# Fused attention, gated layer and gated convolution on one core: a new up operand, a new issue order and work for GpSimd

## The reference

```python
w = softmax(weight_gen, axis=-1)                      # 8 heads, 7 taps
x = sum_k w[..., k] * x_padded[s + k]                 # causal window of 7 tokens, per head of 24 channels
# layer 1
xk = mu_k * x + (1 - mu_k) * x_prev;  xr = mu_r * x + (1 - mu_r) * x_prev
v = relu(xk @ w_k) ** 2 @ w_v                         # 192 -> 1024 -> 192
y = sigmoid(xr @ w_r) * v
# layer 2
h = relu(y @ w_in)                                    # 192 -> 1024
c = conv_w[0] * h[s-1] + conv_w[1] * h[s] + conv_w[2] * h[s+1]
out = (h * sigmoid(c)) @ w_out                        # 1024 -> 192
```

## Time and profile before

| | us |
|---|---|
| median of 3 runs | 737.31 |
| profiled execution, whole | 737.71 |
| its span, first to last instruction | 735.9 |
| PE busy | 696.3 (95%) |
| DVE busy | 681.4 (93%) |
| ACT busy | 648.5 (88%) |
| POOL busy | 3.6 |

### The profile page before, as it was taken

One profiled execution on the slowest core, in us unless ns is written; L12 is line 12 of the kernel. 1 busy time (PEld: TensorE's weight loads), 2 busy tenths in 40 slices (PEclk: granted clock), 3 DMA queues, 4 the chain that ended last, 5 costly groups with the idle time before them and its releaser, 6 DMA issues.

```text
span 735.9 us, 10798 instructions
## 1 busy us (share of the span) xinstructions
PE 696.3 (95%) x3531; PEld 590.7 (80%) x3531; DVE 681.4 (93%) x1057; ACT 648.5 (88%) x1351; POOL 3.6 (0%) x9
## 2 busy tenths in 40 slices
PE   0788999999999999999999999999999999999995
PEld 0677988888888888888888887888888888888984
DVE  7999999999999999998999999999999999786776
ACT  3788999899989989898989889898998989897985
POOL 1000000000000000000000000000000000000000
PEclk9999999999999999999999999999999999999999
DMA  6701101010102001010101101010200101000000
GB/s 157 231 16 40 55 12 54 16 55 22 54 1 71 5 22 55 22 53 23 55 1 28 48 23 53 23 54 0 76 1 23 54 22 44 22 1 1 22 23 21
DMA packets 9053, 28.76 MB, mean 39 GB/s; under 512 B 1038, under 2 KB 4136, under 8 KB 8870
## 3 DMA queue, kind: packets, MB, share of 16 engines
q1 hardware_dynamic: 8840, 28.05, 11.6%
q10 hardware_dynamic: 158, 0.03, 0.0%
HBM read 21.69 MB, written 6.39 MB: 38 GB/s over the span
## 4 chain that ended last, share of the span: by engine, by line
PE 75%; DVE 18%; issue 4%; ACT 1%; DMA 1%; SPq 0%; DVEq 0%; ACTq 0%
PE up L320 32%; PE od L436 20%; PE dn L384 4%; PE dn L400 4%; PE dn L407 4%; PE dn L404 4%; PE dn L403 4%; DVE att L830 3%; PE dn L406 3%; DVE prod L818 3%; DVE cv L927 3%; DVE cv L937 2%; PE mid L291 1%; DVE kq_lo L894 1%; DVE gat L946 1%
## 5 line engine op out<-in xcount | busy, mean ns | idle before, releaser
L436 PE MATMUL od<-wo_sb,gat 128*128 128x192 f32 x1040 | 188.9, 329 | 6.4 <-DVE gat L946 6.3
L436 PEld LDWEIGHTS od<-wo_sb,gat 128*128 128x128 f32 x1040 | 173.8, 191 | 17.7 <-DVE gat L946 5.4
L927 DVE SCALAR_TENSOR_TENSOR cv<-h,prm,cv 128x512 f32<-128x512 f32 (+2 forms) x144 | 98.4, 693 | 19.9 <-ACT cv L606 19.7
L894 DVE TENSOR_TENSOR kq_lo<-ksq,kq_hi 128x512 fp32r<-128x512 f32 (+2 forms) x144 | 89.3, 632 | 14.3 <-ACT kq_hi L572 13.8
L937 DVE SCALAR_TENSOR_TENSOR cv<-h,prm,cv 128x512 f32<-128x512 f32 (+2 forms) x144 | 98.3, 693 | 0.4
L606 ACT ACTIVATE cv<-h,prm 128x512 f32<-128x512 f32 (+2 forms) x144 | 97.0, 675 | 0.0
L818 DVE TENSOR_TENSOR prod<-xin,wgt 128x768 f32<-128x768 f32 (+2 forms) x108 | 95.6, 886 | 1.0
L830 DVE TENSOR_TENSOR att<-att,prod 128x768 f32<-128x768 f32 (+2 forms) x108 | 95.4, 883 | 0.0
L946 DVE TENSOR_TENSOR gat<-h,cv 128x512 f32<-128x512 f32 (+2 forms) x144 | 90.6, 631 | 0.4 <-ACT cv L613 0.2
L597 ACT ACTIVATE h<-up 128x512 f32<-128x512 f32 (+2 forms) x144 | 79.9, 556 | 11.3 <-PE up L320 10.0
L613 ACT ACTIVATE cv<-cv 128x512 f32<-128x512 f32 (+2 forms) x144 | 83.7, 584 | 6.0 <-DVE cv L937 5.3
(11 more groups left out here) (111 smaller groups left out, 1351.6 us busy)
## 6 DMA issues: line engine op xcount, KB each, us to landing
xin<-in_x SPq DMA_DIRECT2D x14, 960.0 KB, 4.7
out<-o_sb SPq DMA_DIRECT2D x14, 384.0 KB, 2.3
wgt<-in_weight_gen SPq DMA_DIRECT2D x1, 1288.0 KB, 6.2
h<-in_moe_w_v SPq DMA_DIRECT2D x1, 768.0 KB, 4.5
wo_sb<-in_moe_w_out SPq DMA_DIRECT2D x1, 768.0 KB, 8.0
xin<-in_x SPq DMA_DIRECT2D x1, 768.0 KB, 4.1
h<-in_moe_w_k SPq DMA_DIRECT2D x1, 512.0 KB, 5.1
h<-in_moe_w_k SPq DMA_DIRECT2D x2, 256.0 KB, 5.6
```

The source lines that it names most:

```text
L436: mm = nc.tensor.matmul(o, lhs, wo_sb[:, c, :], start=(c == 0 and b % 2 == 0), stop=(c == NC - 1), skip_group_check=(b % 2 == 1))
L894: nc.vector.tensor_tensor(ring(kq_lo, c, n), ring(ksq, c, n), ring(kq_hi, c, n).bitcast(F32), ALU.subtract).then_inc(kql_ok, 1)
L927: nc.vector.scalar_tensor_tensor(o, win(w, c, -1), prm[:, 3 + c:4 + c], o, ALU.mult, ALU.add)\
```

## The change

- **Second up layer.** `small_copy`, `add_small`, the shift matrix and the tile `small` are gone. The weights `wr` are now 256 columns wide, with channels 128 to 191 twice, so `r_part` gives the gate in both halves of `dn1`, and `y_mult` multiplies both halves (128 rows instead of 64). `y_hi_part` has a third instruction: part 2 casts all 128 rows into `y2_s`, part 3 casts rows 0 to 63 into `y2_t`, whose rows 64 to 127 get the low part of the upper half. The fourth product of `up2` takes `y2_s`, the fifth `y2_t`; rows 64 to 127 of the weights repeat rows 0 to 63 (in `wi2_lo` they hold a cast of the weight itself), and the product sums the halves.
- **Softmax** in four parts of 448, 672, 1120 and 1456 elements. In parts 1 to 3 GpSimd does the difference and the product; DVE keeps maximum, sum, plus 1e-9 and reciprocal.
- **GpSimd** makes the low parts of `w_in` (1024 columns at a time) and the wrapped columns at the end, by halves of the chunks.
- **Ends.** Slot 0 and the last slot are apart: window NG-1 takes the last slot too and has three slots, window NG has one. ACT leaves out `carry` of window NG-1.
- **Loads.** `w_r` is loaded with six DMAs instead of three, and the softmax weights of part 1 are loaded ahead of `w_in`.
- **Order.** `step(i)` is written anew on PE, ACT and DVE; the numbers of the arguments say nothing, since each engine has its own offset.

```diff
-            nc.gpsimd.memset(small[0:D2, :].bitcast(F32), 0.0).then_inc(small_zero, 1)
+            def split_wi(n):
+                rows = (P, D2)[n]
+                pool.wait_ge(w_cast, 3 + n)
+                nc.gpsimd.tensor_tensor((wi_lo, wi2_lo)[n][0:rows, :], raw_w(2 + n, 0, rows),
+                                        (wi_hi, wi2_hi)[n][0:rows, :].bitcast(F32), ALU.subtract).then_inc(wi_split, 1)
+            def softmax_differences(n):
+                lo, hi = SM_PARTS[n]
+                pool.wait_ge(sm_max, n)
+                nc.gpsimd.tensor_tensor(wgt_rows(lo, hi), wgt_rows(lo, hi), vals(hi - lo)[1], ALU.subtract)\
+                    .then_inc(sm_sub, 1)
+            def softmax_quotients(n):
+                lo, hi = SM_PARTS[n]
+                pool.wait_ge(sm_exp, n + 1)
+                pool.wait_ge(sm_rec, n)
+                nc.gpsimd.tensor_tensor(wgt_rows(lo, hi), wgt_rows(lo, hi), vals(hi - lo)[1], ALU.mult).then_inc(sm_ok, 1)
+            for n in range(2):
+                half = slice(n * HALF, (n + 1) * HALF)
+                pool.wait_ge(h_free, NC * n_windows(NG - 1) - (HALF if n == 0 else 0))
+                nc.gpsimd.memset(h3[:, half, AFTER + PPB - 1:AFTER + P:PPB], 0.0).then_inc(wrap_fix, 1)
+                nc.gpsimd.tensor_copy(part_of(half, AFTER, 0), part_of(half, ALONE, 1)).then_inc(h_wrap, 1)
...
-                terms = ((w_hi, a_hi), (w_lo, a_hi), (w_hi, a_lo), (w2_hi, a2), (w2_lo, a2))
+                terms = ((w_hi, a_hi), (w_lo, a_hi), (w_hi, a_lo), (w2_hi, a2), (w2_lo, b2))
...
-            def add_small(g):
...
-                nc.tensor.matmul(dn[1][0:D2, 0:n], shift[:, :], small[:, 0:n], start=False, stop=True,
-                                 skip_group_check=True)\
-                  .then_inc(sum_done, 1)
...
-                    nc.scalar.activation(y2_s[0:D2, 0:n], y2[:, 0:n], ACT.Copy).then_inc(yhi_ok, 1)
+                    o, rows = (y2_s, P) if part == 2 else (y2_t, D2)
+                    nc.scalar.activation(o[0:rows, 0:n], y2[0:rows, 0:n], ACT.Copy).then_inc(yhi_ok, 1)
...
-        SM_ENDS = [0, FIRST[3] + 1, FIRST[6] + 1, FIRST[9] + 1, FIRST[13] + 1, TPP + 1]
+        SM_ENDS = [0, FIRST[3] + 1, FIRST[6] + 1, FIRST[11] + 1, TPP + 1]
...
-            dve.wait_ge(h_free, NC * n_windows(NG))
-            dve.wait_ge(h_keep, NC)
-            nc.vector.tensor_copy(h3[:, :, 2 * P:3 * P - 1], h3[:, :, KEEP + P + 1:KEEP + 2 * P]).then_inc(h_wrap, 1)
-            nc.vector.tensor_copy(h3[:, :, KEEP + 1:KEEP + P], h3[:, :, P:2 * P - 1]).then_inc(h_wrap, 1)
```

More of the change, by code:

```diff
@@ L526, in xr_hi_part @@
                     nc.scalar.activation(xr2_s[D2:P, 0:n], xkr2[D2:P, 0:n], ACT.Copy).then_inc(xrhi_ok, 1)
-            def small_copy(g):
-                if not group(g):
-                    return
-                act.wait_ge(d_done, NC * g + NC)
-                if not eq(g, 0):
-                    act.wait_ge(sum_done, g)
-                n = size(g) * P
-                nc.scalar.activation(small[D2:P, 0:n], dn[1][D2:P, 0:n], ACT.Copy).then_inc(small_ok, 1)
             def y_hi_part(g, part):
@@ L633, in carry @@
             def carry(w, c):
-                if not window(w):
+                if not window(w) or eq(w, NG - 1):
                     return
@@ L771, in _ @@
+                z_carry(i - 6)
+                k_relu(i - 6, 0)
+                first_tap(i - 7, 4)
+                gate_sigmoid(i - 7, 1)
+                k_square(i - 6, 0)
+                k_relu(i - 6, 1)
+                k_cast(i - 6, 0)
+                k_relu(i - 6, 2)
+                o_copy(i - 8, 0)
+                if i == 6:
+                    cast_wv()
+                o_copy(i - 8, 1)
+                k_square(i - 6, 1)
+            for i in range(3, NG + 9):
                 step(i)
-            act.wait_ge(wrap_fix, 2)
+            act.wait_ge(h_keep, NC)
@@ new lines, in step @@
+                if i == 6:
+                    split_wk(1)
+                k_lo(i - 6, 0)
+                conv_after(i - 7, 3)
+                att_add(i - 5, 2)
+                att_mult(i - 5, 4)
+                k_lo(i - 6, 1)
+                conv_before(i - 7, 4)
+                k_lo(i - 6, 2)
+                if i == 6:
+                    split_wv()
+                att_add(i - 5, 3)
+                gate(i - 7, 1)
+                att_mult(i - 5, 5)
+                att_mult(i - 5, 6)
@@ new lines, in step @@
+                k_lo(i - 6, 3)
+                softmax_front(i - 3)
+                conv_after(i - 7, 4)
+                k_lo(i - 6, 4)
+                gate(i - 7, 2)
+                conv_before(i - 7, 5)
+                att_add(i - 5, 4)
+                k_lo(i - 6, 5)
+                gate(i - 7, 3)
+                att_add(i - 5, 5)
+                k_lo(i - 6, 6)
+                if i == 5:
+                    params()
+                k_lo(i - 6, 7)
+                gate(i - 7, 4)
+                conv_before(i - 7, 6)
@@ new lines, in step @@
+                att_add(i - 5, TAPS - 1)
+                conv_after(i - 7, 5)
+                y_mult(i - 6, 1)
+                y_mult(i - 6, 2)
+                conv_after(i - 7, 6)
+                if i == 5:
+                    split_wk(0)
+                y_lo_part(i - 6, 1)
+                y_lo_part(i - 6, 2)
+                conv_before(i - 7, 7)
+                att_mult(i - 4, 0)
+                gate(i - 7, 5)
+                conv_after(i - 7, 7)
+                att_mult(i - 4, 1)
```

491 lines of the change are left out of this document (229 added, 262 removed).

## The result

The changed kernel takes 745.25 us (median of 4 runs, 744.3 to 746.02); the kernel before, run beside it, 737.32. The ratio is 1.011, with a 95% interval of 1.009 to 1.0122. The forecast was 728.5 us with a range of 723 to 745: the sign was wrong, and the time lies just above the range. The profiled execution has a span of 742.5 us, 6.6 more than before; it was the shortest of the four runs (744.3), so the traces show 1.3 us less of the loss than the medians.

The account below looks back on a forecast made before the run. PE was taken to bound 12 to 14 of 18 groups, DVE the start, a DVE and ACT chain the end. From 737.7 us, -3.7 - 1.6 - 2.3 - 1.5 = -9.1 gave 728.6; forecast 728.5, range 723 to 745.

Parts of the forecast that it names:

- Step 5: GpSimd's own time: eight operations of 7.7 to 23 us in all, taken to cost nothing beside DVE's work.
- Rival A: Start and middle: DVE stands still while GpSimd reads SBUF, so the moved work comes back on DVE; 742 us, chance 0.3.
- step 2: Softmax in the middle groups: a group absorbs about 4.8 us, and 0.3 us of stall is left; -1.6 us.
- Step 3: The start: DVE is rid of 4.3 us of work, against a later arrival of `w_in`; -2.3 us.
- The walk: The start's new DVE order gone through with old spacings: last low part of y of group 1 ends at 59.0.
- step 4: The end: 33.4 against 32.5 us, but two `down2` chunks behind the last `down1` bring it 2.6 earlier; -1.5 us.
- The wait of 3 us for `kq_hi`: The start: DVE was to wait about 3 us near 32, with ACT's casts of `w_in` ahead of k chunks.
- Step 1: `add_small` goes: a shorter PE in all 18 groups by product spacing, with 0 taken for stalls; -3.7 us.
- B: All groups: the new order stalls PE, y half a microsecond late in 14 groups; 735.5 us, chance 0.12.
- C: The start brings nothing, `w_in` late and the order no better, its term +2; 733 us, chance 0.08.

Follow-up runs that it names:

- experiment 6: The kernel before with `add_small` removed and `w_r` loaded by six DMAs, old order, everything on DVE: 737.27 us, 0.9998 of the kernel before.
- experiment 1: The changed kernel with all of GpSimd's arithmetic (softmax and the split of `w_in`) back on DVE, end copies left on GpSimd: 739.76 us, 1.0026 of the kernel before.
- experiment 2: The changed kernel with only the softmax differences and quotients back on DVE, the split of `w_in` left on GpSimd: 741.5 us, 1.0058 of the kernel before.
- experiments 4 and 7: The changed kernel with GpSimd's arithmetic on DVE and five softmax parts, 735.39 us; that kernel with 11 additional GpSimd instructions of 768 elements, 734.72 us, single run.

## Why the prediction was wrong, by its steps

**Step 5 failed:** "Beside DVE's work they cost nothing in this sum." In its place the traces show 15.7 us in which DVE stood still, for work that takes DVE itself 10.1, and the medians show 5.5 us more than with that work on DVE. It was also what the forecast stood on: with GpSimd at nothing, DVE is 10 us lighter. Rival A had this mechanism, its place in the start and the middle, and its sign, and 742 us for the time; it got 0.3 because no row showed the two engines together. The missing row was no evidence against it. That A comes so near the time is in part luck: it stood on the same 4.8 us of step 2, and took off 2.4 us for a wait of DVE that did not come. Its range is also worked out a little wide: by its own terms 0.9, 2.2 and 2.7 ns give 734.3, 745.4 and 749.7 us, where the text has 733.5, 746 and 751. GpSimd's rate was inside the bounds: 2.0 to 2.2 ns an element for the quotients (1456 in 3.02 us), up to 2.6 for the splits, 20.3 us for all where the page GPSIMD Engine Reference of the Trainium skill (Performance versus the Vector engine) led to an estimate of 18.8; part of the excess is GpSimd's own waiting for DVE, since the two instructions of 1120 elements took 3.54 and 2.43 us.

**Step 2 failed in its rule.** "So a group absorbs about 4.8" was read from a group of before in which both halves of a softmax part fell. The new order puts the halves into two groups that follow each other, and each takes in some 2.5 us: 2.4 us of first half of the part of 1008 cost nothing (41.50 us), 3.7 and 4.2 us of second half cost 1.05 and 1.64 over 41.48. So larger parts were no gain. The two groups of the part of 1456 are 43.1 and 46.4 us in the changed kernel, where no group was to be above 42. By themselves, all on DVE, the larger parts cost 4.4 us; the term was -1.6, with GpSimd's help in it.

**Step 3, the start.** The walk had the last low part of y of group 1 end at 59.0 us. It starts at 66.97, and with nothing on GpSimd at 64.69, against 65.84 before. In the changed kernel there are waits that the walk left out: PE for `xk_hi` (2.1 us), for `wv_parts` (1.6) and for `kq_lo` (2.7), ACT for DVE. What each is worth in the time is not shown. Up to group 4 the changed kernel lost 3.1 us where -2.3 was forecast: 3.2 are GpSimd's, and 2.3 the part of 1120, whose quotient falls there; -2.4 is the rest, and of that 1.9 is group 2, which I put down to step 4. So with GpSimd's part and the larger parts taken out, the new order is worth 0.5 us in the start. The wait of 3 us for `kq_hi` was not there in the changed kernel (0.7 at most), nor with nothing on GpSimd (0.42 us, up to 33.7); in the old order (experiment 6) it was 2.5.

**Step 1: the mechanism right, the size off.** Steady groups take 41.48 us, 0.2 less than 41.68, as the spacing says. But this was counted for all 18 groups, though the prediction's own rows show DVE full from 20 to 106 us. In the old order it made 2.0 us, not 3.7.

**Step 4: nearly right.** The step's 33.4 us count from DVE's first product of y, its 32.5 from 0.3 us earlier; counted as 33.4 is, the kernel before has 32.2. By that measure it is 33.5 us in the changed kernel: DVE's last gate of window NG-1 ends after 19.8 us (19.1 in the text), the next tap comes 2.5 us later (3.2), the eight rounds take 7.15 (7.4), and the rest 4.1 (3.7). In the 19.8 us three of DVE's taps are too long, by 0.23, 0.34 and 0.34 us, beside GpSimd's copies of the wrapped columns: 0.9 us of standstill where the step gave the move no cost and rival A said that the end gives 0. No run has these copies back on DVE. From the start of the last product of `down1`, as in the table, it is 33.9 us, against 32.8 before. The chunks of `down2` that moved behind are, as I read it, what shortens group 2, 27.36 us against 29.25: -1.9 where -2.6 was said. Together -0.8 for -1.5.

**Rivals B and C.** B is out: PE is full in every steady group (41.50 of 41.50). C, that the start gives nothing, was half of the truth, hidden under A: 0.5 us of step 3 is left.

The sum by runs: 5.5 us for GpSimd's arithmetic and 4.4 for the larger parts, less 2.0 for all the rest (737.4 to 735.4), make the 7.9 us by which the changed kernel is slower.

## What to carry to other kernels

Before work is moved from DVE to GpSimd, ask whether DVE's instructions at that time read two operands from SBUF. If they do, the move costs DVE most of the length of the GpSimd instruction instead of its own: here 15.7 of 20.3 us, 1.5 times as much as doing the work. A memset, and work beside DVE instructions that read one operand from PSUM, cost DVE nothing here, and what falls into a group with DVE time to spare costs no time. A helper job on an engine with 2.5 us to spare in a group should be cut until each piece, in the group where it falls, is smaller than that; seven parts were worth 2.3 us over five, and five 4.4 over four. And a rival with a known mechanism is not made unlikely by the lack of a row: where the two engines have never run together in the trace, its chance is that of the mechanism.

## What was not expected of the hardware

- GpSimd is stopped as well: a copy of 768 elements took 2.12 us while two DVE instructions ran through, and 0.88 where DVE waited. Its busy time in the profile holds such waits.
- A GpSimd addition of 768 elements took 1.82 to 1.89 us, a copy 0.88, a memset 0.74: the second operand costs 0.94 to 1.01, more than the first and the write together.
- PE's clock. The second half of the part of 1456 elements leaves PE idle. In experiment 1's kernel PE has one gap of 2.05 us (363.70 to 365.75), and in the table of stretches the granted clock (third column from the right) falls after it, in this stretch and the next:

```profile
364.00:368.00 4.00, 2.25 (x7) 1.85 (x8) 4.00 (x7) 2.12 (x4) 0.00 (x0) 0.84 0.01 2
368.00:372.00 4.00, 4.00 (x14) 2.88 (x13) 4.00 (x7) 3.74 (x7) 0.00 (x0) 0.73 0.02 4
372.00:376.00 4.00, 4.00 (x18) 3.10 (x18) 4.00 (x7) 4.00 (x10) 0.00 (x0) 1.00 0.64 202
```

In experiment 2's kernel, with the same instructions in that group and one gap of 2.06 us (365.78 to 367.84), the clock stayed at 1.00 (2.4 GHz):

```profile
364.00:368.00 4.00, 1.94 (x12) 1.56 (x11) 3.96 (x6) 0.81 (x2) 0.00 (x0) 1.00 0.00 0
```

That group took 45.68 us in the one and 44.64 in the other, so the spell in which part of the time was granted at 1.2 GHz goes with 1 us on top of the stall. Over the whole group PE is idle for 2.12 us in the one and 2.19 in the other. Why the clock fell in the one and not in the other these runs don't show. In the changed kernel it fell too (0.96 over that group), there after a gap of 2.79 us. It also fell in its start, after a gap of 1.65 us, and there it costs little: the kernels of experiments 4 and 7 are the same up to group 4 but for one memset at 4 us, one has such a spell and the other none, and the last `down1` of group 0 starts at 41.4 and at 41.0 us.
